# Other order and queues for the first loads of a kernel of attention and two mixtures of experts, and a first batch of (states @ w1) that is copied on chip

## The reference

```python
B, H, S, Ns, D = (4, 8, 512, 32, 64)          # x: [B,H,S,D], state: [B,H,Ns,D]
scores = scale * x @ state^T;   a  = softmax(scores);   xread = a @ state
scores2 = scale * state @ x^T;  a2 = softmax(scores2);  sread = a2 @ x
x = concatenate([xread, sread], axis=2) -> rows [B*(S+Ns), H*D]
# first MoE: all experts, weights P from 8 rounds of row and column sums
for e in range(8):
    out += P[:, e:e+1] * (relu(x @ w1[e]) @ w2[e])
# second MoE: the one expert of the highest logit
out[mask] = gate_w[mask, None] * eom[mask, e, None] * (relu(x[mask] @ w1[e]) @ w2[e])
```

## Time and profile before

| | us |
|---|---|
| median of 3 runs | 1619.7 |
| lowest and highest | 1616.66 and 1619.8 |
| the profiled execution | 1622.05 |
| its span | 1620.3 |
| TensorE busy in it | 1556.9 |
| VectorE, ScalarE, GpSimd busy | 632.5, 516.3, 53.6 |

### The profile page before, as it was taken

The page is one execution under the profiler, slowest core; times in us unless marked ns, Lnnn a source line. Parts: engine busy times, 40 slices in busy tenths (PEclk is TensorE's granted clock), DMA queues, the critical chain, the costliest instruction groups (busy, mean ns, idle before and its releaser), DMA issues.

```text
span 1620.3 us, 20524 instructions
## 1 busy us (share of the span) xinstructions
PE 1556.9 (96%) x7288; PEld 1258.0 (78%) x7289; DVE 632.5 (39%) x1010; ACT 516.3 (32%) x873; POOL 53.6 (3%) x73
## 2 busy tenths in 40 slices
PE   4899999999999999999999999999999996999997
PEld 3687868877877887788778877877888885888885
DVE  4545464334333523342333334333422226535221
ACT  4433343233223413331332234223312222435121
POOL 1000000000000000000000000000000001111110
PEclk9889999999999999999999999999999987999998
DMA  7530134134213412330332034112310233444110
GB/s 195 158 85 27 53 112 155 34 103 124 60 53 104 124 33 78 109 115 12 104 124 85 27 105 130 52 55 95 100 32 27 91 130 130 146 147 138 39 41 15
DMA packets 111908, 143.57 MB, mean 89 GB/s; under 512 B 33040, under 2 KB 65808, under 8 KB 111824
## 3 DMA queue, kind: packets, MB, share of 16 engines
q1 hardware_dynamic: 107104, 131.70, 25.8%
q0 software_dynamic: 3200, 9.70, 1.8%
q10 hardware_dynamic: 1520, 1.05, 0.2%
HBM read 99.93 MB, written 43.25 MB: 88 GB/s over the span
## 4 chain that ended last, share of the span: by engine, by line
PE 92%; DVE 3%; DMA 2%; ACT 1%; issue 1%; SPq 0%; ACTq 0%; POOL 0%; DVEq 0%; POOLq 0%
PE PS L834 15%; PE PS L835 14%; PE PS L836 14%; PE PS L820 7%; PE PS L822 7%; PE PS L821 7%; PE PS L600 3%; PE PS L982 2%; PE PS L1005 2%; PE PS L1007 2%; PE PS L983 2%; PE PS L984 2%; PE PS L1006 2%; PE PS L590 1%; PE PS L992 1%; PE PS L874 1%
## 5 line engine op out<-in xcount | busy, mean ns | idle before, releaser
L834 PE MATMUL PS<-w2h,hTh 128*128 128x512 f32 x1024 | 408.8, 399 | 0.0
L835 PE MATMUL PS<-w2l,hTh 128*128 128x512 f32 x1024 | 400.0, 391 | 0.0
L836 PE MATMUL PS<-w2h,hTl 128*128 128x512 f32 x1024 | 399.4, 390 | 0.0
L1460 DVE SCALAR_TENSOR_TENSOR hTl<-PS,hTh 128x512 fp32r<-128x512 f32 x256 | 177.0, 691 | 559.3 <-ACT hTh L1132 559.1
L1132 ACT ACTIVATE hTh<-PS 128x512 fp32r<-128x512 f32 x256 | 153.0, 598 | 672.0 <-PE PS L822 672.0
L834 PEld LDWEIGHTS PS<-w2h,hTh 128*128 128x128 f32 x1024 | 192.8, 188 | 61.9 <-DVE hTl L1460 18.9
L836 PEld LDWEIGHTS PS<-w2h,hTl 128*128 128x128 f32 x1024 | 192.6, 188 | 41.1
L835 PEld LDWEIGHTS PS<-w2l,hTh 128*128 128x128 f32 x1024 | 192.9, 188 | 37.2
L820 PE MATMUL PS<-aTh,swh 128*128 128x512 f32 x512 | 201.5, 394 | 9.2 <-DVE swl L1456 8.0
L822 PE MATMUL PS<-aTh,swl 128*128 128x512 f32 x512 | 199.8, 390 | 0.0
L821 PE MATMUL PS<-aTl,swh 128*128 128x512 f32 x512 | 199.8, 390 | 0.0
(11 more groups left out here) (225 smaller groups left out, 1586.2 us busy)
## 6 DMA issues: line engine op xcount, KB each, us to landing
sw_rows<-swout SPq DMA_DIRECT2D x128, 256.0 KB, 2.4
swraw<-sw_rows SPq DMA_DIRECT2D x512, 64.0 KB, 2.2
raw<-in_moe_w SPq DMA_DIRECT2D x10, 2048.0 KB
w1raw<-in_moe_w SPq DMA_DIRECT2D x69, 256.0 KB, 3.1
w2raw<-in_moe_w SPq DMA_DIRECT2D x64, 256.0 KB, 2.8
x_in<-in_x SPq DMA_DIRECT2D x16, 256.0 KB, 4.6
x_rows<-acc SPq DMA_DIRECT2D x16, 256.0 KB, 2.7
w1raw<-in_moe_w ACTq DMA_DIRECT2D x3, 256.0 KB, 6.9
```

The lines of the kernel that those rows point to most:

```text
L834: mm(PS[:, 4 + j, :], hTh[:, i % 2, ts], w2h[:, fc, :], start=(fc == 0), stop=False)
L835: mm(PS[:, 4 + j, :], hTh[:, i % 2, ts], w2l[:, fc, :], start=False, stop=False)
L836: last = mm(PS[:, 4 + j, :], hTl[:, i % 2, ts], w2h[:, fc, :], start=False, stop=(fc == CF - 1))
L1460: V.scalar_tensor_tensor(out=hTl[:, i % 2, :], in0=PS[:, 0, :], scalar=0.0, in1=hTh[:, i % 2, :].bitcast(F32), op0=ALU.max, op1=ALU.subtra ...
```

## The change

It has four parts.

1. **States.** One DMA brings all states to `st_in` (rows: 4 heads of 32 states; 8 groups of 64 elements), first on SyncE. VectorE copies each group beside itself (`st_twice`), TensorE does 8 transposes instead of 16, and ScalarE copies the diagonal blocks into `stT_bd`, which VectorE has cleared (128x1024 instead of `st_bd`'s 128x2048).
2. **Loads.** Of batch 0's four loads of x two are issued by ScalarE, ahead of everything, and two by SyncE. `w1` chunks 0 and 2 follow on ScalarE, 1, 3 and the `w2` loads on SyncE between other work. The loads of batches 1, 2 and 3 are issued by GpSimd, behind waits for `w1h(2)`, for the copies of chunks 0 to 3 with hidden(0), and for the first `states_read`. The subtractions of chunks 0 to 3 move from GpSimd to VectorE.
3. **Copy on chip.** For the first expert `direct_sw(k)` copies batch 0's 32 rows of each chunk by a DMA from `first_out` or `swout` straight into `swraw`. Quarters 0 to 3 aren't loaded from DRAM. The stores go on, for batches 1 to 3. `first_out` holds the first four buffers, so that the ring `swout` is free longer.
4. **Order beside the steps.** The turns of batch 1 move from `attention_first` to the place behind chunk 5 and to steps 0 to 2, and the rest of the attention is dealt out anew over steps 2 to 16. In a step, ScalarE does `high_sw` ahead of `attention_beside`. The `w1` chunks 8 and 9 are split in step 16 instead of steps 0 and 1.

```diff
-            load_x(0)
-            for fc in range(W2_RING):
-                load_w2(fc)
-            load_x(1)
+            sp.dma_start(st_in[:, :, 0, :], state.rearrange("b (g r) n d -> (r n) (b g) d", r=4)).then_inc(state_loaded, 16)
+            load_x_rows(sp, 0, 0)
+            load_x_rows(sp, 0, 1)
+            load_w1(1)
             load_w1(3)
+            direct_sw(0)
+            load_w2(0)
             load_w1(4)
-            store_sw(0)
+            direct_sw(1)
+            direct_sw(2)
+            load_w2(1)
+            direct_sw(3)
             load_w1(5)
-            for k in range(1, CD):
+            for k in range(CD):
                 store_sw(k)
-            for q in range(2):
-                load_sw(q)
...
+            def direct_sw(k):
+                half, c = k // CD, k % CD
+                for u in range(2):
+                    g = 2 * k + u
+                    sp.wait_ge(sw_out[u], k + 1)
+                    src = first_out[0:NS, g, :] if g < OUT_RING else swout[0:NS, g % OUT_RING, :]
+                    row = (c % 2 * 2 + u) * NS
+                    dst = swraw[row:row + NS, 2 * half:2 * half + 2, c // 2, :]
+                    ins = sp.dma_start(dst, src.rearrange("p (q f) -> p q f", q=2))
+                    ins.then_inc(sw_direct[half], 16)
...
# GpSimd
-            for m in range(CD):
-                pool.wait_ge(w1_hi, m + 1)
-                pool.tensor_tensor(w1l[:, m % 2, :], w1raw[:, m % W1_RING, :], w1h[:, m % 2, :].bitcast(F32),
-                                   ALU.subtract).then_inc(w1_lo, 1)
+            pool.wait_ge(w1_hi, 3)
+            for j in range(J):
+                load_x_rows(pool, 1, j)
+            pool.wait_ge(sw_first, 16 * OUT_RING)
+            pool.wait_ge(sw_direct[0], 16 * 2 * CD)
+            pool.wait_ge(h_done, 1)
+            for j in range(J):
+                load_x_rows(pool, 2, j)
+            pool.wait_ge(sr_done, 1)
+            for j in range(J):
+                load_x_rows(pool, 3, j)
...
# ScalarE
-            act.wait_ge(zeroed, 1)
-            for r in range(4):
-                dst = st_bd[r * NS:(r + 1) * NS, :, :].rearrange("n (k u) m -> n k u m", u=2)
-                src = state.rearrange("b (g r) n d -> r n (b g) d", r=4)[r]
-                act.dma_start(dst[:, :, r // 2, (r % 2) * DH:(r % 2 + 1) * DH], src).then_inc(state_loaded, 16)
-            for m in range(W1_RING):
+            load_x_rows(act, 0, 2)
+            load_x_rows(act, 0, 3)
+            for m in (0, 2):
...
             def high_sw(q):
-                act.wait_ge(sw_loaded[q % SW_RING], 64 * (q // SW_RING + 1))
+                if q < SW_RING:
+                    act.wait_ge(sw_direct[q // 2], 16 * 2 * CD)
+                else:
+                    act.wait_ge(sw_loaded[q % SW_RING], 64 * (q // SW_RING))
...
# TensorE, behind hidden(0) and ahead of the loop
             states_chunk(4, 2)
-            pe.wait_ge(xT_ready, 8)
             states_chunk(5, 6)
+            pe.wait_ge(x_loaded[1], 16 * J)
+            pe.wait_ge(sub_done, 2)
+            x_turn(1, 0, 1)
...
# TensorE, attention_beside, steps 3 and 4 as they are now
+                elif i == 3:
+                    states_scores(1, 0, 1)
+                    states_scores(1, 1, 2)
+                    pe.wait_ge(gates_loaded, 48)
+                    states_read(0, 3)
+                elif i == 4:
+                    scores_turn(1, 0, 1)
+                    scores_turn(1, 1, 2)
+                    pe.wait_ge(x_loaded[2], 16 * J)
+                    x_turn(2, 0, 3)
```

More of the change, by code:

```diff
@@ L133, in attention_then_two_moes @@
         lgT, _ = place("lgT", [2 * E, N], F32, xT_at)
-        st_bd, _ = place("st_bd", [P, PAIRS, P], F32, h_at)
+        st_in, _ = place("st_in", [P, B * G, 2, DH], F32, h_at)
+        first_out, _ = place("first_out", [P, OUT_RING, BANK], F32, acc_at + 4 * J * D)
         a1, _ = place("a1", [P, J * H * NS], F32, sT_at)
@@ L231, in attention_then_two_moes @@
         sw_out = [sem(f"sw_out{u}") for u in range(2)]
+        st_twice = sem("st_twice")
+        sw_first, sw_direct = sem("sw_first"), [sem(f"sw_direct{half}") for half in range(2)]
         s_step, s_relu, sT_done, sT_hi, sT_lo = sem("s_step"), sem("s_relu"), sem("sT_done"), sem("sT_hi"), sem("sT_lo")
@@ L329, in x2_rows_of, with load_x_rows @@
             return dst[b * ROWS:b * ROWS + S, :].rearrange("(p j) d -> j p d", j=J)[j]
+        def load_x_rows(queue, b, j):
+            src = x[b].rearrange("h (p j) d -> j p h d", j=J)[j]
+            queue.dma_start(x_in[:, (b + 2) % 3, j, :].rearrange("p (h d) -> p h d", h=H), src).then_inc(
+                x_loaded[b] if b else x0_loaded[j], 16)
         @block.sync
         def _(sp):
[L334 to L338, removed]
             def load_w1(m):
@@ L364, in load_sw @@
                 half = quarter // 2
-                stores = 4 * CD * e + (4 * CD if half else 2 * CD)
+                if e == 0:
+                    sp.wait_ge(sw_first, 16 * OUT_RING)
+                stores = 4 * CD * e + (4 * CD if half else 2 * CD) - OUT_RING
                 for s in range(OUT_RING):
@@ L635, in attention_first @@
                 pe.wait_ge(pool_made, MADE_FIRST)
-                pe.wait_ge(state_loaded, 16 * 4)
-                for q in range(PAIRS):
-                    last = tr(PS[:, 4 + q // 4, (q % 4) * P:(q % 4 + 1) * P], st_bd[:, q, :], ident[:, :])
+                pe.wait_ge(state_loaded, 16)
+                pe.wait_ge(st_twice, 1)
+                for k in range(B * G):
+                    last = tr(PS[:, 4 + k // 4, (k % 4) * P:(k % 4 + 1) * P],
+                              st_in[:, k, :, :].rearrange("p u d -> p (u d)"), ident[:, :])
                 last.then_inc(stT_done, 1)
@@ L1174, in attention_first @@
                     keep_sw(3, u, 2 + u)
-                for c in range(CD):
-                    copy_x(1, c, (0, 1, 6, 7)[c])
-                high_w1(4)
                 copy_weights(0, 0, 4)
@@ L1259, in attention_beside @@
+                    high_w1(8)
+                    high_w1(9)
                 elif i == LOGITS_STEP + 1:
@@ L1513, in attention_first @@
                 low_sw(0)
-                dve.wait_ge(w1_lo, CD)
                 low_w1(4)
-                low_w1(5)
                 low_w2(0)
                 low_h(0)
+                max_states(0)
+                low_sw(1)
+                low_w1(5)
                 dve.wait_ge(sw_out[1], 4)
                 keep_sw(4, 3)
+                keep_sw(5, 7)
                 low_w1(6)
-                keep_sw(5, 7)
                 low_w1(7)
                 low_w2(1)
-                low_sw(1)
+                sum_states(0)
             def attention_beside(i):
```

383 lines of the change are left out of this document (190 added, 193 removed).

## The result

| | us | ratio to before, 95% interval |
|---|---|---|
| changed kernel, median of 5 runs | 1608.47 (1605.67 to 1611.17) | 0.9937 [0.9924, 0.9950] |
| before, median of 5 runs beside it | 1619.02 (1616.66 to 1619.80) | |
| changed kernel again, with the first experiments on order | 1608.07 | 0.9925 [0.9908, 0.9941] |
| and with the last experiments | 1608.31 | 0.9917 [0.9899, 0.9934] |

The change made the kernel faster by about 0.6 to 0.8%. The prediction was 1603.0, a gain of 16.7 us; the gain of the profiled executions is 10.9 (1622.05 to 1611.17), and the time lies in the range of 1596 to 1613. All that follows is about the 5.8 us between.

What follows compares the result with a forecast made beforehand. TensorE, busy 96%, was taken as the bound, so only its idle or low-clock stretches could give time. 12.2 - 0.3 + 9.3 - 4.5 = 16.7 us off 1622.05 gave 1605.35, as median 1603.0; range 1596 to 1613, the forecast's own 1596 to 1609.

Steps and rivals of the forecast that it cites:

- Point 1, the first scores: Start of TensorE's first scores: 17.20 us before, 12.8 forecast, a gain of 4.4, bounds 11.5 and 15.
- To the turn of a1: First scores to TensorE's turn of a1: scores 1.94 us, then 8.5 from copying s, reaching 23.35.
- its bounds for the clock: TensorE's clock falling once or twice between 21.5 and 37.5 us: 4.5 us lost, bounds 0 and 7.
- From there to hidden(0): Turn of a1 to hidden(0): 3.4 us, reaching 26.8 instead of 38.99, a gain of 12.2; on-chip copy landing in 2.0.
- (a): Each x load costs GpSimd 3.5 to 7 us, so x(1) is waited for before step 0: 1609, chance 0.12.
- (c): VectorE stops GpSimd while it runs, x(1) lands near 38, 5 us lost: 1608, chance 0.08.
- From hidden(0) to the end of output(1): TensorE's stretch: 19.95 us with new w1l waits before chunks 5 and 6; with 2.45 owed, 22.4 against 22.1.
- point 3: End of output(1), TensorE's second part of step 1: 61.06 us before; its stretch from hidden(0) counted minus 0.3.
- After point 3: Behind output(1): a 3.1 us wait and low-clock losses of 3.4 and 2.8 go, 9.3 us back.
- (b): GpSimd's x loads cost by the piece, 8.2 us each, so batches land late: 1625, slower, chance 0.06.
- (d): New waits missed in steps 2 to 17, 3 us each for two or three: 1609 to 1612, chance 0.08.
- (e): Small packets bound the start, on-chip copy no sooner than the round trip, 12.2 us gone: 1615, chance 0.04.

Runs made afterwards that it cites:

- c1_changed: The changed kernel itself, unedited, run again beside the first experiments on order: 1608.07 us, ratio 0.9925 to the kernel before.
- e8: Changed kernel with fourteen more transposes on TensorE ahead of the states' transposes: 1607.14 us, ratio 0.9916 to the kernel before.
- e10: Changed kernel with batch 1's four x loads issued by SyncE ahead of the first on-chip copy, none by GpSimd: 1608.29 us, ratio 0.9915.
- e2: Changed kernel with GpSimd's four x loads of batch 1 issued sooner, behind w1h(0) instead of w1h(2): 1605.05 us, ratio 0.9895.
- e5: Changed kernel with chunk 5's w1 split, a copy out of PSUM and w1h(6) moved ahead on VectorE and ScalarE: 1604.85 us, ratio 0.9906.
- e11: e9 with ten more unread products of 512 columns on TensorE ahead of hidden(0): 1603.46 us, ratio 0.9896 to the kernel before.
- e1: Changed kernel with GpSimd's four x loads of batch 1 issued behind the landing of the eight on-chip copies: 1607.42 us, ratio 0.9910.
- e9: Changed kernel with the edits of e2 and e5 together: 1606.95 us, ratio 0.9903 to the kernel before.
- e4: Changed kernel without the on-chip copy: batch 0's four quarters go through DRAM again, stored and loaded back: 1611.54 us, ratio 0.9935.
- e3: Changed kernel with SyncE's first two w2 loads moved behind the last on-chip copy: 1607.71 us, ratio 0.9908 to the kernel before.
- c2_changed: The changed kernel itself, unedited, run again beside the last experiments: 1608.31 us, ratio 0.9917 to the kernel before.

## Why the prediction was right, and what it had too large

**Point 1, the first scores: right.** Predicted 12.8, measured 13.15. The states' transposes began at 5.41, the `stTl` subtractions took 1.41 for two without GpSimd's beside them (before 1.70 for one):

```profile
10.00 1.41 DVE L1536 TENSOR_TENSOR stTl<-stT_bd,stTh 64x512 fp32r<-64x512 f32 x2 [4.74 <-ACT stTh L1191]
```

**To the turn of a1: 23.35 predicted, 25.71 measured, 2.4 late.** 0.35 of it is point 1, 1.74 the two pairs of scores at the lower clock (3.68 instead of 1.94). Where these and the twelve transposes ahead ran at full clock the turn came at 23.60 (c1_changed), 23.49 (e8) and 23.32 (e10), as predicted; where only the scores did, it came at 24.35 to 24.39 (e2, e5 and e11). The prediction took the pair's duration from the earlier trace rows, one run at the full clock, and its bounds for the clock began only at 21.5.

**From there to hidden(0): 3.4 predicted, 7.86 measured, 4.4 late. This is the step that failed.** The sentence "if it lands in 2.0 like the load into the same tile", with 3.2 as its bound, was worth 4.0 of the 4.4. The row it came from the earlier trace rows was measured with DMA engines that were busy 0.55 in that window, and 0.46 in the two us of that load (35.5 to 37.5); the change itself made them busy 1.00 there. The store of 3.17 in the same rows flew at 0.89 to 1.04 (27 to 31), so the row with the traffic was there, as the bound and not as the forecast. The prediction weighed GpSimd's loads in every way but this one: what they cost GpSimd and when they land, in rivals (a) to (c), and SyncE's freed queue. It did not ask whom the bytes hold up. By the Trainium skill ("DMA: Bandwidth & Descriptors", Issuing engines are not separate DMA queues), DMAs of SyncE, ScalarE and GpSimd run on the same 16 engines and interleave; e1, e2 and e9 agree: the last copy landed in 2.46, 2.1 and 2.3 where these loads were elsewhere. The other 0.4 is a second, smaller slip, of the issue. The prediction had the last copy issued 0.05 to 0.45 ahead of the turn of a1; it was issued 0.4 to 0.6 behind it in the changed kernel, e1, e2 and e9, since each issue of an on-chip copy takes SyncE 0.6 and a `w2` load stands between. So even with GpSimd's loads elsewhere the stretch took 4.12 to 4.50 (e1, e2, e9), not 3.4.

**From hidden(0) to the end of output(1): right.** Predicted 19.95 and 4.5 for the clock, 24.45; measured 33.57 to 57.93, 24.36. Both new waits for `w1l` are there, ending at 40.43 and 46.60. They are shorter than the 3.35 and 2.6 of the walk (2.53 and 1.69), since the slow matmuls ahead fill a part of them; that the sum is right is not luck, for chunks 5 and 6 start 6.86 and 13.03 behind hidden(0), where the walk with its terms for the clock gives 6.75 and 13.15. The clock was low in hidden(0), in most of hidden(1) and in the first seven of output(0)'s twelve matmuls.

**At point 3** that leaves 61.06 - 57.93 - 2.45 = 0.7 gained where 7.4 was predicted (-0.3 and -4.5 with 12.2). The difference of 6.7 is the lateness of hidden(0), 6.8.

**After point 3: right.** 9.3 predicted, 10.9 - 0.7 = 10.2 measured, so 0.9 of the 6.7 came back here. Batch 0's states are read at full clock, in 3.79 beside 7.09 in the earlier trace rows:

```profile
67.55 3.79 PE L619 MATMUL PS<-a2T,x_in 128*128 128x64 f32 x32
```

**What was luck.** That the time lies even in the forecast's own range, 1596 to 1609, is luck in part. Its slow side held 2 us for the start, 1.2 for the copies and 2.5 more for the clock. Up to the turn of a1 2.4 were lost and from there to hidden(0) 4.4, more than the first two held; but the clock's 2.5 weren't needed behind hidden(0), and 0.9 came back behind point 3.

**The rivals.** (a), (b) and (c) fell: GpSimd issues a load in 0.88 to 1.12 us (3.81 for four, the lower end that I had from the gather; I took 2 to 3), beside a VectorE that was 1.97 of 2 us busy. x was never waited for in the steps. (d): no new wait above 0.4 us in steps 2 to 17. (e) had the right place, "the on-chip copy lands no sooner than the round trip", and too much of it: e4 puts the round trip 3.1 to 3.8 us behind the copy.

## What to carry to other kernels

A duration of a DMA holds for the traffic that it was measured in. Where a change moves transfers, write down for each stretch what is in flight, and cost every DMA on the critical path, a small one on chip as well, with that traffic beside it; a queue of another engine frees the issue slots, not the DMA engines. Bulk loads go where no small copy is waited for, here 4 us earlier (e2). And where one late landing hides a second one, undoing the first alone gives little back: look at what each ring buffer waits for before adding two gains up.

## What the runs showed of the hardware

- A copy of 64 KB from SBUF to SBUF took 2.0 to 3.0 us to land with little beside it (all eight copies of e1 ahead of hidden(0)). The last of them took 5.07 to 6.37 with GpSimd's loads of 256 KB each among SyncE's other transfers (e3, c2_changed), and a later one 7.14 (e9).
- GpSimd issued a plain load of 1024 pieces of 256 bytes in 0.88 to 1.12 us, much like a gather of 128 rows. SyncE took 0.6 for an on-chip copy of 32 partitions.
- The same loads look unlike in the records of the two queues. From 12 to 36 us, packets, MB and share of 16 engines of the queue that carried them, in c2_changed:

```profile
q0 software_dynamic: 320, 1.05, 19.1%
```

  and in e10, with all that SyncE moved:

```profile
q1 hardware_dynamic: 6688, 5.02, 75.5%
```

  320 packets for 1.05 MB are 3.3 KB a packet; in e10, 4493 of its packets are under 512 bytes, in c2_changed 365. The 19.1% of 24 us is 4.6 us of all 16 engines for the 1.05 MB, 229 GB/s. Whether long packets are what a small copy queues behind was not tried by itself.
- The point at which TensorE's pace doubles in the opening differs between runs of one program (twelve transposes in 1.53 or in 2.82 us), and it can do so with nothing but transposes run. With the slow ones the turn of a1 came 2.1 to 2.7 us later, so it is likely one cause of the changed kernel's spread, 1605.2 to 1612.2 us in 15 runs.
